# Four tasks of token mixing in one step of the second batch's attention

## What is computed

```
scores = (q @ k.T) / 8;  thresh = max(scores) - tau
attn = exp(where(scores >= thresh, scores, -1e9) - max);  attn /= sum;  x = attn @ v      # 4 batches, 8 heads
h = x.T @ U @ V                  # token mixing, rank 32
u = x + h.T
u = u + relu(u @ w_ch1) @ w_ch2  # channel network, 512 -> 2048 -> 512
logits, gate = u @ w_gate, u @ w_local;  e = expert by logits and gate, row by row
out = p[e] * (relu(u @ w1[e]) @ w2[e])
```

## Time and profile before

| | |
|---|---|
| median of three runs | 1092.53 us |
| the profiled execution's own time | 1092.55 us |
| its span in the profile | 1090.7 us |
| PE busy | 1048.8 us, 96% |
| DVE, ACT, POOL busy | 512.3, 471.1, 369.6 us |
| granted TensorE clock, mean | 0.998 |

### The profile page before, as it was taken

The page is one execution under the profiler, slowest core; times in us unless marked ns, Lnnn a source line. Parts: engine busy times, 40 slices in busy tenths (PEclk is TensorE's granted clock), DMA queues, the critical chain, the costliest instruction groups (busy, mean ns, idle before and its releaser), DMA issues.

```text
span 1090.7 us, 19998 instructions
## 1 busy us (share of the span) xinstructions
PE 1048.8 (96%) x7142; PEld 918.9 (84%) x7142; DVE 512.3 (47%) x1022; ACT 471.1 (43%) x914; POOL 369.6 (34%) x339
## 2 busy tenths in 40 slices
PE   6999899999999999999999999999989999999997
PEld 5666889999788999978799997999978888888885
DVE  4675554445444444444444443322275533255642
ACT  5676543544545344454533432423114533245531
POOL 4454322624421542633154254079511111111111
PEclk9999999999999999999999999999999999999999
DMA  7887152516344251625233222342066444164611
GB/s 162 192 181 194 39 122 65 141 56 161 103 120 104 89 132 50 169 65 155 58 107 83 77 78 77 142 136 78 1 213 199 146 133 146 40 204 142 214 64 41
DMA packets 110729, 127.52 MB, mean 117 GB/s; under 512 B 67229, under 2 KB 67229, under 8 KB 110624
## 3 DMA queue, kind: packets, MB, share of 16 engines
q1 hardware_dynamic: 104480, 114.54, 36.9%
q0 software_dynamic: 3600, 11.01, 3.1%
q10 hardware_dynamic: 2544, 0.59, 0.3%
HBM read 88.16 MB, written 10.22 MB: 90 GB/s over the span
## 4 chain that ended last, share of the span: by engine, by line
PE 82%; SPq 6%; DVE 4%; ACT 4%; issue 3%; POOL 1%; DMA 0%; POOLq 0%; ACTq 0%; DVEq 0%
PE mlp_banks L732 16%; PE mlp_banks L740 15%; PE p_down L1434 11%; PE p_up L1434 11%; PE aux L690 6%; PE score_banks L666 5%; PE score_banks L673 5%; PE score_banks L740 2%; PE score_banks L732 2%; PE p_turn L1461 2%; PE mlp_banks L715 2%; DVE stat L986 1%; PE p_x L1428 1%; PE aux L633 1%; PE mlp_banks L722 1%
## 5 line engine op out<-in xcount | busy, mean ns | idle before, releaser
L838 ACT ACTIVATE ex<-score_banks,stat 128x576 f32<-128x576 f32 x132 | 97.8, 741 | 165.7 <-DVE stat L986 165.7
L512 POOL CAST w_hi<-stage 128x1024 fp32r<-128x1024 f32 x64 | 66.6, 1041 | 302.5 <-PE mlp_banks L732 249.8
L995 DVE SCALAR_TENSOR_TENSOR ex<-score_banks,stat,ex 128x576 f32<-128x576 f32 x132 | 107.7, 816 | 107.4 <-ACT stat L842 105.7
L517 POOL TENSOR_TENSOR w_lo<-stage,w_hi 128x1024 fp32r<-128x1024 f32 (+1 forms) x70 | 154.3, 2206 | 4.8
L732 PE MATMUL mlp_banks<-u_hi,w_hi 128*128 128x256 f32 (+1 forms) x448 | 138.6, 309 | 3.9 <-DVE u_lo L1031 2.2
L740 PE MATMUL mlp_banks<-hid_hi,w_hi 128*128 128x256 f32 (+1 forms) x448 | 138.4, 309 | 2.7 <-ACT u_hi L887 2.1
L732 PE MATMUL mlp_banks<-u_hi,w_lo 128*128 128x256 f32 (+1 forms) x448 | 132.4, 296 | 0.0
L740 PE MATMUL mlp_banks<-hid_hi,w_lo 128*128 128x256 f32 (+1 forms) x448 | 132.4, 296 | 0.0
L732 PE MATMUL mlp_banks<-u_lo,w_hi 128*128 128x256 f32 (+1 forms) x448 | 132.4, 295 | 0.0
L740 PE MATMUL mlp_banks<-hid_lo,w_hi 128*128 128x256 f32 (+1 forms) x448 | 132.3, 295 | 0.0
L986 DVE TENSOR_REDUCE stat<-score_banks 128x1 f32<-128x576 f32 x132 | 99.2, 752 | 23.2 <-PE score_banks L666 17.0
(11 more groups left out here) (264 smaller groups left out, 2045.1 us busy)
## 6 DMA issues: line engine op xcount, KB each, us to landing
stage<-in_moe_w_ch SPq DMA_DIRECT2D x64, 512.0 KB, 3.7
w_raw<-in_moe_w SPq DMA_DIRECT2D x64, 512.0 KB, 5.2
q_tiles<-q_parts SPq DMA_DIRECT2D x30, 320.0 KB, 4.2
q_tiles<-q_parts SPq DMA_DIRECT2D x60, 160.0 KB, 4.2
k_tiles<-k_parts SPq DMA_DIRECT2D x60, 144.0 KB, 3.5
raw_q<-in_q SPq DMA_DIRECT2D x32, 128.0 KB, 2.5
raw_v<-in_v SPq DMA_DIRECT2D x32, 128.0 KB, 2.7
raw_k<-in_k SPq DMA_DIRECT2D x28, 128.0 KB, 2.7
```

The costliest lines, as they stand in the source:

```text
L512: nc.gpsimd.tensor_copy(w_hi[:, n % RING], stage[:, n % 2]).then_inc(w_upper, 1)
L517: last = nc.gpsimd.tensor_tensor(w_lo[:, n % RING, cols], stage[:, n % 2, cols], w_hi[:, n % RING, cols].bitcast(F32), ALU.subtract)
L838: nc.scalar.activation(ex_of(n), score_of(n), ACT.Exp, bias=stat[:, n % 4, 0:1], scale=-1.0).then_inc(exp_done, 1)
L995: nc.vector.scalar_tensor_tensor(out=ex_of(n), in0=score_of(n), scalar=stat[:, n % 4, 1:2], in1=ex_of(n), op0=ALU.is_le, op1=ALU.mult, acc ...
```

## The change

Two numbers tables change; no instruction is added or removed. The second batch's steps (36 to 71) got 0, 1, 2, 2, ... tasks; now they get 0, 1, 4, 2, ... So the four `mixed` tasks of the first half stand in one step (38), and from there every task stands earlier by two tasks, which is one step. In the third batch two of the four steps with three tasks get two, so that the new plan is one task ahead after step 92 and falls in with the old one at step 103.

```diff
-THREES = {2: (15, 20, 25, 30), 3: (15, 17, 20, 22, 25, 27, 30, 32)}
+THREES = {2: (15, 25), 3: (15, 17, 20, 22, 25, 27, 30, 32)}
...
-            want = min(at, 2)
+            want = (0, 1, 4)[at] if at < 3 else 2
```

## The result

| | before | after |
|---|---|---|
| median of five runs | 1092.53 us (1092.07 to 1094.24) | 1097.4 us (1097.0 to 1098.5) |
| profiled execution | 1092.55 us, span 1090.7 | 1097.00 us, span 1095.3 |
| ratio of medians | 1 | 1.0040, 95% interval 1.0029 to 1.0050 |

The kernel became slower by 4.9 us, 4.45 us by the two profiled executions. 1096.1 was predicted, range 1094.4 to 1099.0.

A forecast was written before the change was run, and what follows sets the result against it. PE bounds the kernel (busy 96% of the span, 82% of the chain), so only its gaps count: -0.7 first border, +3.2 token mixing, +1.0 rest of second border, +3.5 on 1092.55, so 1096.1 us; range 1094.4 to 1099.0.

The forecast's parts named there:

- First border: Steps 37 to 46: PE gaps filled by the moved tasks, less new waits, 0.7 us gained.
- The three waits for `u_lo`: Step 38 on PE: third and fourth `mixed` and first `hidden` wait 1.66, 0.39 and 0.98 us, 3.03 against 3.26.
- The wait in front of `hidden` in step 46: Step 46 on PE: 0.74 us by starts goes, as the task moves into step 45 behind products with the values.
- Token mixing: Step 73, second batch: PE waits for DVE's last write of x, a gap of 3.2 us, bounds 2.9 to 3.4.
- Rest of the second border: Steps 71 to 84 without the token mixing: waits grow by 1.0 us in all, bounds -0.5 to +2.
- The `rows` task in step 77: Step 77 on PE: `rows` uses the logits' bank and waits for DVE's sums, +1.4 us.
- the wait in step 71: Step 71 on PE: the wait at 276.22 grows by 0.3 us, with a `rows` task where the logits stood.
- that of step 80: Step 80 on PE: the second `mixed` waits 1.15 us where 0.86 was waited, +0.3.
- Stacking of pair 8: POOL and SP: last transfer at about 266, landing near 270, scores due about 273; free. Rival of lateness: 1098.5, chance 0.05.
- The clock: Rival: clock halves in the token mixing's new gap, 0 to 4.4 us, taken as 2.2, giving 1098.3; chance 0.20.
- the third case: Rival: only the token mixing counts, rest of border evens out, +2.5, 1095.1 us; chance 0.62 together with the forecast.
- Catching up: Rival: the pause lets ACT and DVE clear a backlog, waits from 299.43 to 343.80 go, 1091.0 us; chance 0.05.

The follow-up runs named there:

- first border alone: Changed kernel's steps 36 to 38, earlier plan from step 68, single tasks of steps 63 and 67 behind `turn`, against before: 1092.49 us, ratio 0.9983.
- second border alone: Earlier kernel's steps at the first border, three tasks in steps 63 and 67, changed plan from step 68, against before: 1098.13 us, ratio 1.0038.
- The exchange of two neighbours: Changed kernel with step 73's tasks exchanged, `channel` first, then token mixing behind `turn`: 1094.2 us, ratio to before 1.0001.
- the two filled kernels: Changed kernel with 24 or 12 unused transposes ahead of the second batch's token mixing: 1096.66 and 1096.09 us, ratios to before 1.0025 and 1.0018.

## Why the prediction was right, point by point

- **First border, -0.7 predicted.** Measured -0.65 (first border alone) and -0.57 (after less second border alone). The three waits for `u_lo` came where they were put: 1.66, 0.39 and 0.98 by starts were predicted, and by starts the first two measured 1.66 and 0.39 (1.42 in the row for the first), the third 0.88 in the row and some 1.1 by starts. The wait in front of `hidden` in step 46 is gone.
- **Token mixing, +3.2 predicted.** The row says 3.20. By starts it is 289.40 - 284.75 = 4.65 less the 1.29 at which PE would have been free, 3.36; 4.53 less 1.29 was predicted. The step from the last write to PE's start took 0.26 in place of 0.14, which is all of the difference. The exchange of two neighbours agrees with this price: 2.3 of wait and 1.7 of clock less a new wait of 0.8 give the 3.2 that it measured.
- **Rest of the second border, +1.0 predicted: mis-sized.** What remains of +4.74 is 4.74 + 0.65 - 3.36 - 1.71 = +0.3. Read the other way, the waits of 0.15 and more from 262 us to the third batch's token mixing add up to 5.89 before (eleven) and to 6.62 after without the token mixing's own (nine): +0.7. So it is between +0.3 and +0.7, within the bounds given (-0.5 to +2). The `rows` task in step 77 waits for the sums of the logits as predicted (1.23, or 1.39 by starts, for 1.4), the wait in step 71 grew by 0.22 for 0.3, that of step 80 by 0.25 for 0.3. That of step 83 shrank by 0.08 only; the smaller one in the step before went as predicted. Two were not in my list: a wait of 0.34 at 374 us went, and `gate` in step 69 starts 0.77 behind its scores (266.12 to 266.89), 0.24 more than the four scores take (0.53, 284.75 to 285.28).
- **Stacking of pair 8, free with 3 to 4 us of margin.** The last transfer was issued at 264.81 for the 266 predicted (answers to rows 11), and no scores wait for `q_tiles` or `k_tiles`:

```profile
264.81 0.60 SPq L350 DMA_DIRECT2D k_tiles<-k_parts  x1
```

- **The clock, a rival at 0.20 with 0 to 4.4 us.** It happened in the profiled execution and costs 1.71, near the 2.2 taken. The case allowed for twice the token mixing's length, but the half clock lasted 3.4 of its 6.07 us. The forecast without it, 1096.1, was too high in the rest by 0.3 to 0.7 and too low by the clock, and so came within 1.3 us of the median, 0.9 of the profiled execution. That closeness is in part luck. Without the clock the distances give -0.65 + 3.36 + 0.3 = +3.0, halfway between the forecast's 3.5 and the 2.5 of the third case, in which the rest of the border evens out. The chance was too small. I had weighed holes of 1.3 to 1.7 us that kept the clock against it, but those show only that such a hole can be harmless, not that it is; in the last stage a hole of 1.32 lost the clock in four executions.
- **The range's low end.** 1094.4 doesn't follow from its words: 2.9 and half of -0.7 + 1.0 are +3.05, which makes 1095.6. 1094.4 is near what 2.9, -0.7 and the lower bound of the rest, -0.5, add up to (+1.7, 1094.3).
- **Catching up** is refuted: the waits behind the token mixing didn't shrink by microseconds, 306.54 to 347.21 still hold 0.78, 1.23, 0.36, 0.64, 0.96 and 0.77, 4.74 in all where before had 4.04 in eight.

What stays open: at what moment within a hole the clock decides, and so whether other executions of the changed kernel lose it. Only one of its five has a trace. Their mean granted clocks are 0.997 (the profiled one), 0.996, 0.996, 0.996 and 0.998. An estimate: 3.4 us at the half lower the mean of 1095 us by 0.0016, so the last one probably had no such fall, and the others one or more, at a place that the mean doesn't tell. Yet the last took 1097.08 us and the profiled one 1097.00, so that whole times don't single out the clock's price. The ratios of the two filled kernels are 1.6 and 2.4 us below the changed kernel's, but they are to executions of before with a median 1.0 us higher; the medians themselves are 0.7 and 1.3 us lower. The clock's share is shown in the traces and not in the medians. The wait's share doesn't hang on it.

## What to carry to other kernels

A task that is moved earlier in an engine's queue, up to a point where its last input isn't there yet, costs the whole distance to that input, since everything behind it waits too; look for the last writer of its input, and put one task that is ready ahead of it. Filling a gap with tasks that share two banks fills it with waits for the banks. Of a new hole on TensorE count the hole and, as a second term with a chance of its own, the work behind it at half the clock; two traces of the same work, one with and one without the fall, tell the two apart. How much idle filling it takes to keep the clock these runs don't show.

## What the runs showed of the hardware

- The granted clock fell after the work had begun again. PEclk was 1.00 at 289.4, when the token mixing started, 0.78 in the slice from 290 and 0.50 from 291 to 294. Ten matmuls that need 4.36 us took 6.07, with 3.4 us of them at the half.
- At the three places followed here it fell behind holes of 3.20 (two kernels), of 2.12, in four of twelve executions of 1.32, and in three of twelve of 0.96 and 0.79 together. It stayed behind holes of 2.55, 1.68, 0.89, 0.54 and 0.37 at the token mixing, and behind the same short holes of the other two places in all other executions.
- One fall costs 1.2 to 1.7 us, and 3.1 in the one case in which the half clock lasted about twice as long. That is as much as the hole itself in the smaller cases, and 0.1 to 0.3% of this kernel. Comparisons of two single executions can differ by that with no change in between; the distance between two instructions around the place in question leaves out the falls elsewhere.
